# A dynamic convolution and a SwiGLU layer on one Trainium2 core: the first tile's work divided anew among the engines

## What is computed

```python
w = softmax(weight_gen, axis=-1)                     # 4 x 4096 x 8 heads x 7 taps
x_unf[b, s, k] = x_pad[b, s + k]                     # 6 rows of zeros ahead of each sequence
y = einsum('bshk,bskhg->bshg', w, x_unf)             # 4 x 4096 x 192, 24 columns to a head
xn = y / sqrt(mean(y * y, -1) + 1e-6) * rms_g        # 16384 x 192
g, val = xn @ w_gate, xn @ w_val                     # 192 x 1536 each
out = (g * sigmoid(g) * val) @ w_out                 # 1536 x 192
```

## Time and profile before

| | |
|---|---|
| median of 3 runs | 1282.7 us |
| the profiled execution | 1281.68 us |
| its span in the profile | 1279.7 us |
| PE, matmuls | 1261.2 us busy, 99% |
| PEld, weight loads | 1180.4 us, 92% |
| DVE | 1002.0 us, 78% |
| ACT | 662.6 us, 52% |
| POOL | 44.7 us, 3% |

### The profile page before, as it was taken

The page is one execution under the profiler, slowest core; times in us unless marked ns, Lnnn a source line. Parts: engine busy times, 40 slices in busy tenths (PEclk is TensorE's granted clock), DMA queues, the critical chain, the costliest instruction groups (busy, mean ns, idle before and its releaser), DMA issues.

```text
span 1279.7 us, 32479 instructions
## 1 busy us (share of the span) xinstructions
PE 1261.2 (99%) x13544; PEld 1180.4 (92%) x13544; DVE 1002.0 (78%) x1516; ACT 662.6 (52%) x1426; POOL 44.7 (3%) x75
## 2 busy tenths in 40 slices
PE   8999999999999999999999999999999999999998
PEld 7988999999999899999989999999999999999997
DVE  7998888878787887888877777877877877877643
ACT  4554555565446555445564455554455554455543
POOL 1000000000000000000000000000000000000000
PEclk9999999999999999999999999999999999999999
DMA  9011321211211212212212112111122122121010
GB/s 292 40 43 27 97 67 44 69 58 56 62 47 56 69 45 69 57 38 69 69 45 68 47 50 69 53 61 57 44 64 69 45 69 57 39 69 39 14 38 14
DMA packets 19734, 76.29 MB, mean 60 GB/s; under 512 B 3212, under 2 KB 4876, under 8 KB 19464
## 3 DMA queue, kind: packets, MB, share of 16 engines
q1 hardware_dynamic: 18764, 72.78, 18.8%
q10 hardware_dynamic: 828, 1.47, 0.5%
HBM read 38.06 MB, written 12.58 MB: 40 GB/s over the span
## 4 chain that ended last, share of the span: by engine, by line
PE 90%; DVE 4%; issue 2%; ACT 2%; DMA 1%; ACTq 0%; POOL 0%; DVEq 0%
PE up_ps L796 57%; PE out_ps L836 22%; PE out_ps L840 10%; DVE h L683 1%; DMA raw<-in_moe_w_val 1%; DVE prod L224 1%; DVE y L226 1%; DVE h_lo L703 1%; PE up_ps L745 1%; ACT silu L469 1%; ACT L469 0%; ACT L449 0%; PE up_ps L750 0%; DMA taps<-in_weight_gen 0%; DVE last L635 0%
## 5 line engine op out<-in xcount | busy, mean ns | idle before, releaser
L796 PE MATMUL up_ps<-xT,w_hi 64*128 64x512 f32 x4608 | 779.7, 390 | 4.3 <-DVE h L683 3.5
L796 PEld LDWEIGHTS up_ps<-xT,w_hi 64*128 64x128 f32 x4608 | 481.2, 184 | 51.4 <-issue 6.7
L796 PE MATMUL up_ps<-xT,w_lo 64*128 64x512 f32 x2304 | 476.1, 387 | 0.0
L836 PE MATMUL out_ps<-wo,h_hi 64*128 64x384 f32 x3072 | 456.0, 354 | 5.5 <-DVE last L635 1.6
L484 ACT ACTIVATE h_hi<-h 128x512 fp32r<-128x512 f32 x384 | 242.4, 631 | 338.8 <-DVE h L683 332.2
L683 DVE TENSOR_TENSOR h<-up_ps,silu 128x512 f32<-128x512 f32 x384 | 264.4, 688 | 194.0 <-ACT silu L469 191.7
L840 PE MATMUL out_ps<-wo,h_lo 64*128 64x192 f32 x3072 | 413.3, 247 | 0.0
L469 ACT ACTIVATE silu<-up_ps 128x512 f32<-128x512 f32 x384 | 228.5, 595 | 238.9 <-PE up_ps L796 232.2
L836 PEld LDWEIGHTS out_ps<-wo,h_hi 64*128 64x128 f32 x3072 | 322.6, 184 | 11.2 <-DVE last L635 2.4
L840 PEld LDWEIGHTS out_ps<-wo,h_lo 64*128 64x128 f32 x3072 | 327.3, 187 | 3.7
L703 DVE TENSOR_TENSOR h_lo<-h,h_hi 128x512 fp32r<-128x512 f32 x384 | 263.1, 685 | 34.9 <-ACT h_hi L484 34.6
(11 more groups left out here) (75 smaller groups left out, 301.5 us busy)
## 6 DMA issues: line engine op xcount, KB each, us to landing
x_buf<-in_x SPq DMA_DIRECT2D x30, 960.0 KB, 4.7
xT<-xT SPq DMA_DIRECT2D x90, 256.0 KB, 3.8
result<-last SPq DMA_DIRECT2D x32, 384.0 KB, 2.3
taps<-in_weight_gen SPq DMA_DIRECT2D x1, 3136.0 KB, 20.7
raw<-in_moe_w_gate SPq DMA_DIRECT2D x3, 384.0 KB, 8.6
raw<-in_moe_w_val ACTq DMA_DIRECT2D x3, 384.0 KB, 10.4
last<-in_moe_w_out SPq DMA_DIRECT2D x1, 1152.0 KB, 18.0
x_first<-in_x SPq DMA_DIRECT2D x2, 384.0 KB, 7.4
```

Source lines behind the costliest of these rows:

```text
L796: mm = nc.tensor.matmul(ps[:, banks, :], w[rows, s, cols], xT[rows, t, s, part, :], start=(at == 0), stop=ends)
L836: nc.tensor.matmul(out_ps[:, j, 0:2 * D], h_hi[rows, g % HB, cols], wo[rows, g, :, :].rearrange("p a d -> p (a d)"), start=(g == 0 and k < ...
```

## The change

- **DMA.** Gate, value and output weights are loaded in halves of columns (blocks), all of half 0 ahead of half 1. The gains come in three transfers instead of five, ahead of the value weights. Each half has its own semaphore.
- **Transposes that nobody reads.** 34 ahead of `sum_first` instead of 50, 34 behind it instead of 30, and 6 new ones (`WAIT_TURNS`) between `turn_x` of tile 0 and the first hidden block.
- **ACT at the start.** `w_high(0, 1)` goes ahead of the squares, `w_high(0, 2)` stays behind them.
- **PE.** The steps of hidden blocks 0 and 1 of tile 0 are interleaved, so that those which need low x come later.
- **POOL** takes the products with the last two taps of tile 1's convolution and their sum (`last_taps`), the low weights of half 1 for s = 0 and 1 (`w_low_pooled`) and those of the output weights' second half (`wo_low_pooled`). ACT scales the raw weights by the gains for it (`raw_times_gains`), since POOL's form is a plain subtraction.
- **DVE** is left with 10 instead of 13 steps in tile 0 and `w_low(1, 2)` alone in half 1; tile 1's squares and scales come one f earlier, and so does `scale_rest(1, 1)`. Four steps of tile 2's division of taps and two products move into f = 9 to 11 of tile 0. At tile 1 `out_low` and `out_add` come at f = 0 instead of 2.

```diff
-        WARM_TURNS, KEEP_TURNS = 50, 30
+        WARM_TURNS, KEEP_TURNS, WAIT_TURNS = 34, 34, 6
...
-        SECOND_DONE = NORM1_DONE + CONV
+        SECOND = CONV - 3
+        SECOND_DONE = NORM1_DONE + SECOND
...
-            def load_w(s):
-                c = CHUNKS[0][s]
-                sp.dma_start(raw[0:DB, s, :], w_gate[c * DB:(c + 1) * DB, :]).then_inc(w_loaded[s], 16)
+            def load_gate(n, s):
+                c, cols = CHUNKS[0][s], slice(n * F // 2, (n + 1) * F // 2)
+                sp.dma_start(raw[0:DB, s, cols], w_gate[c * DB:(c + 1) * DB, cols]).then_inc(w_loaded[n][s], 16)
+
+            def load_out(n):
+                fs = slice(n * FB // 2, (n + 1) * FB // 2)
+                sp.dma_start(raw_out[:, fs, :], w_out_d[:, fs, :]).then_inc(wo_loaded[n], 16)
...
             load_first(0)
-            load_w(0)
+            load_gate(0, 0)
             load_taps(1)
-            load_w(1)
-            load_w(2)
+            load_gate(0, 1)
+            load_gate(0, 2)
             load_first(1)
-            sp.dma_start(raw_out, w_out_d).then_inc(wo_loaded, 16)
+            load_out(0)
+            for s in range(SLOTS):
+                load_gate(1, s)
+            load_out(1)
...
+            def last_taps():
+
+                heads = lambda a: a.rearrange("p (q g) -> p q g", g=G)
+                pool.wait_ge(xfirst_loaded[1], 16)
+                pool.wait_ge(first_mix, NORM1_DONE)
+                for n, product in enumerate((prod_first, prod_pool)):
+                    k = K - 2 + n
+                    nc.gpsimd.tensor_tensor(heads(product[:]), heads(flat(x_first[:, J + k:J + k + J, :])),
+                                            tap_w[:, :, k].unsqueeze(2).to_broadcast([P, J * H, G]), ALU.mult).then_inc(pool_mix, 1)
+                pool.wait_ge(pool_mix, 2)
+                nc.gpsimd.tensor_tensor(prod_first[:], prod_first[:], prod_pool[:], ALU.add).then_inc(pool_mix, 1)
+
+            def w_low_pooled(s):
+                cols = slice(F // 2, F)
+                pool.wait_ge(raw_scaled, s + 1)
+                nc.gpsimd.tensor_tensor(w_lo[:, s, cols], raw[:, s, cols], w_hi[:, s, cols].bitcast(F32),
+                                        ALU.subtract).then_inc(w_lo_pooled, 1)
+
+            def wo_low_pooled():
+                fs = slice(FB // 2, FB)
+                pool.wait_ge(wo_hi_done, 2)
+                nc.gpsimd.tensor_tensor(wo[:, fs, 1, :], raw_out[:, fs, :], wo[:, fs, 0, :].bitcast(F32),
+                                        ALU.subtract).then_inc(wo_lo_done, 1)
+
             inverse_rms(0)
+            last_taps()
...
+            w_low_pooled(0)
...
+            w_low_pooled(1)
...
+            wo_low_pooled()
...
-            load_val(0)
-            act.dma_start(gains[:, 0:1], g_d[0:P, :]).then_inc(gains_loaded, 16)
...
+            with nc.allow_non_contiguous_dma(reason="192 gains, one to a partition"):
+                chunks = g_d.rearrange("(s c) a -> c (s a)", c=DB)
+                act.dma_start(gains[0:DB, :], chunks).then_inc(gains_loaded, 16)
+                act.dma_start(gains[DB:P, 0:SLOTS:2], chunks[:, 1:SLOTS]).then_inc(gains_loaded, 16)
+                act.dma_start(gains[DB:P, 1:2], chunks[:, 0:1]).then_inc(gains_loaded, 16)
+            for n in range(2):
+                for s in range(SLOTS):
+                    load_val(n, s)
...
+            def raw_times_gains(s):
+                cols = slice(F // 2, F)
+                nc.scalar.activation(raw[:, s, cols], raw[:, s, cols], ACT.Copy, scale=gains[:, s:s + 1]).then_inc(raw_scaled, 1)
...
+            w_high(0, 1)
             square(0, 0, range(J))
-            w_high(0, 1)
             w_high(0, 2)
...
-                squares_early, scales_early = {0: 10, 1: 7, 2: 6, 3: 3}.get(T), {0: 11, 1: 8}.get(T)
+                squares_early, scales_early = {0: 9, 1: 7, 2: 6, 3: 3}.get(T), {0: 10, 1: 8}.get(T)
...
-                    if f == 2 and not first:
+                    if f == (0 if T == 1 else 2) and not first:
                         out_low(T - 1)
...
                     if first and f in (1, 2, 3):
                         w_high(1, f - 1)
+                        if f < 3:
+                            raw_times_gains(f - 1)
...
             w_low(0, 0)
+            w_low(0, 1)
             scale_rest(0, 0)
-            w_low(0, 1)
             w_low(0, 2)
...
+                    if n == SECOND - 1:
+
+                        dve.wait_ge(pool_mix, 3)
+                        first_step(NORM1_DONE + n, nc.vector.tensor_tensor(flat(y[:, 1, :, :]), flat(y[:, 1, :, :]),
+                                                                           prod_first[:], ALU.add))
+                        continue
...
-            seconds = [1, 0, 1, 1, 1, 2, 2, 1, 2, 2, 0, 0]
+            seconds = [0, 1, 1, 1, 1, 2, 2, 2, 0, 0, 0, 0]
...
+            steps_early = {0: (None,) * 9 + ((2, 4), (2, 1), (2, 1)),
...
-                        if f in (2, 3, 4):
-                            w_low(1, f - 2)
-                        if f == 7:
-                            wo_low(1)
+                        if f == 4:
+                            w_low(1, 2)
...
-                    if first and f == xf:
+                    if first and f == xf - 1:
                         scale_rest(1, 1)
...
-                if T < 2 and f == 0:
+                if T == 0 and f < 2 or T == 1 and f == 0:
...
                 if first and f == FB // 2:
-                    pe.wait_ge(w_lo_done, 2 * SLOTS)
+                    pe.wait_ge(w_lo_done, SLOTS + 1)
+                    pe.wait_ge(w_lo_pooled, SLOTS - 1)
...
+                    if first and f == 0:
+
+                        hidden(T, t, 0, 0, 7)
+                        hidden(T, t, 1, 0, 4)
+                        hidden(T, t, 0, 7)
+                        hidden(T, t, 1, 4)
+                        continue
...
             turn_x(0, 0, 1)
+            for _ in range(WAIT_TURNS):
+                nc.tensor.transpose(up_ps[:, 0, 0, 0:P], ident[:], ident[:])
```

More of the change, by code:

```diff
@@ L109, in dynconv_swiglu @@
         gains_loaded = sem("gains_loaded")
-        w_loaded = [sem("w_loaded0"), sem("w_loaded1"), sem("w_loaded2")]
-        wo_loaded = sem("wo_loaded")
+        w_loaded = [[sem(f"w_loaded{n}{s}") for s in range(SLOTS)] for n in range(2)]
+        wo_loaded = [sem("wo_loaded0"), sem("wo_loaded1")]
         x_loaded = [sem("x_loaded0"), sem("x_loaded1")]
@@ L127, in dynconv_swiglu @@
         first_mix = sem("first_mix")
+        pool_mix = sem("pool_mix")
+        raw_scaled = sem("raw_scaled")
+        w_lo_pooled = sem("w_lo_pooled")
         y_summed = sem("y_summed")
@@ L361, in _, with load_val @@
             first_exps(0)
-            def load_val(s):
-                c = CHUNKS[1][s]
-                act.dma_start(raw[DB:P, s, :], w_val[c * DB:(c + 1) * DB, :]).then_inc(w_loaded[s], 16)
-            load_val(0)
-            act.dma_start(gains[:, 0:1], g_d[0:P, :]).then_inc(gains_loaded, 16)
-            for s in (1, 2):
-                for m in range(2):
-                    c = CHUNKS[m][s]
-                    act.dma_start(gains[m * DB:(m + 1) * DB, s:s + 1], g_d[c * DB:(c + 1) * DB, :]).then_inc(gains_loaded, 16)
-            load_val(1)
-            load_val(2)
+            def load_val(n, s):
+                c, cols = CHUNKS[1][s], slice(n * F // 2, (n + 1) * F // 2)
+                act.dma_start(raw[DB:P, s, cols], w_val[c * DB:(c + 1) * DB, cols]).then_inc(w_loaded[n][s], 16)
+            with nc.allow_non_contiguous_dma(reason="192 gains, one to a partition"):
[6 more added lines that the diff above has]
+                    load_val(n, s)
             def w_high(n, s):
-                if n == 0:
-                    if s == 0:
-                        act.wait_ge(gains_loaded, 80)
-                    act.wait_ge(w_loaded[s], 32)
+                if n == 0 and s == 0:
+                    act.wait_ge(gains_loaded, 48)
+                act.wait_ge(w_loaded[n][s], 32)
                 cols = slice(n * F // 2, (n + 1) * F // 2)
@@ L638, in _ @@
             second_norm()
-            seconds = [1, 0, 1, 1, 1, 2, 2, 1, 2, 2, 0, 0]
+            seconds = [0, 1, 1, 1, 1, 2, 2, 2, 0, 0, 0, 0]
             steps_other = [2, 1, 2, 2, 1, 1, 1, 1, 2, 1, 2, 1]
-            steps_early = {1: ((2, 2), (2, 2), (2, 1), (2, 2), (2, 2), (2, 2), (2, 2), None, (3, 4), None, (3, 1), (3, 2)),
+            steps_early = {0: (None,) * 9 + ((2, 4), (2, 1), (2, 1)),
[1 row of a table added]
                            2: ((3, 2), (3, 2), (3, 1), (3, 2), (3, 2), (3, 1, 4, 3), (4, 2), (4, 2), (4, 2), None, (4, 2), (4, 2)),
                            3: ((4, 2), (4, 2), (5, 3), (5, 3), (5, 1), (5, 2), (5, 1), None, (5, 2), (5, 1), (5, 2), (5, 2))}
-            steps_done = {2: NORM, 3: 0, 4: 0, 5: 0}
+            steps_done = {2: 0, 3: 0, 4: 0, 5: 0}
             early = {}
-            for T in (1, 2, 3):
+            for T in (0, 1, 2, 3):
```

(13 more changed lines are left out.)

9 lines of the change are left out of this document (7 added, 2 removed), and 1 row of the table steps_early.

## The result

The changed kernel took **1286.3 us** (median of 9 runs, 1285.37 to 1286.87) beside 1282.7 us for the kernel before in 9 runs of the same measurement: 1.0023 times as long, with a 95% interval of 1.0015 to 1.0032. Forecast were 1281.0 us and a gain of 1.7. So the sign is wrong, and the value lies above the range. The profiled execution took 1286.37 us, 4.7 more than the profiled one of before, which lay 1.0 under its median.

A forecast was written before the change was run, and what follows sets the result against it. PE was taken as the bound nearly throughout, with gains only where it falls behind its pace: 2.8 + 1.4 + 1.9 = 6.1 us, less 4.4 for POOL, gives 1.7 off 1282.7, so 1281.0; range 1275.6 to 1285.2.

The forecast's parts named there:

- tile 1's block 4 at 77.0: Start of tile 1's block 4 on PE: 77.0, which is 78.65 less the 1.7 us gain.
- The start: Start of tile 0: `turn_x` at 19.3 against 22.68, 3.4 us sooner; 2.8 us gained by block 4.
- The mechanism of the hold: DVE instructions with two SBUF inputs wait for POOL's instructions that read SBUF, as POOL waits for DVE's; assumed.
- Its price: P, a POOL instruction's time, taken as 1.4 us; 5P - 2.67 = 4.4 us lost ahead of `project(0)`.
- The rival of a high price: POOL's instructions hold DVE in f = 0 and 1 from P = 2.5 up; 1287.4 at 2.7; chance 0.12.
- The clock during the stall: PE's clock while it waits ahead of `project(0)` of tile 0: the prediction had no term for it.
- block 4 of tile 0 at 37.9: Start of tile 0's block 4 on PE, expected at 37.9 if the forecast is right; 36.29 before.
- four slow pairs at the start: First pairs of tile 0 at the low clock: about 1.7 us if not covered, costed at nothing.
- The last POOL instruction … is done well before: POOL's last instruction, and anything PE needs from POOL (block 6, `project(6)`), comes in time; no cost.
- PE stalls in f = 4 to 9, which I have at none: Blocks f = 4 to 9: PE never waits; stalls there would show the forecast wrong.
- The end of tile 0: Block 10's start to tile 1's start: 9.42 us instead of 10.83, 1.4 gained.
- Tile 1: Tile 1's blocks 0 to 3 and `project(0)`: 10.49 us instead of 12.43, 1.9 gained.

The follow-up runs named there:

- run 5: The changed kernel with the low half of the output weights for blocks 6 to 11 back on DVE at f = 7: 1284.75 us, 1.0014.
- run 2: The changed kernel with 40 more unread transposes ahead of `project(0)` of tile 0: 1285.31 us, 1.0022.
- the second kernel of run 9: The changed kernel without POOL's part, squares behind the first `w_hi`, one convolution step at tile 1's f = 0: 1279.83 us, 0.9975.
- runs 3 and 4: 3: changed kernel, POOL held until the second `h_lo`, 1284.46 us. 4: changed kernel without POOL's part, unused memsets and copies added on POOL, 1282.59 us.
- run 6: The changed kernel with 40 unread transposes ahead of `project(0)` and `wo_low(1)` back on DVE at f = 7: 1283.89 us, 1.0003.

## Why the prediction was wrong

The step that failed is the price of POOL's work: the forecast stopped at the wait of `project(0)`, took the work behind it at full speed, and put POOL's sixth instruction at nothing. I forecast tile 1's block 4 at 77.0; the trace has 83.08 (the medians differ by 5.3). The 6.1 us between, step by step:

- **The start**, "19.3 for `turn_x`": 20.03, **0.7 short**. The six pairs of sums ran nearly as forecast, from 7.7 to 15.5. I gave the second `w_hi` until 15.5 and looked only at its own load. But two `w_hi` of 0.94 stand back to back ahead of the squares, and the first could begin only at 14.32, so they end at 16.2. That first start varies from one profiled execution to the next, from 13.75 (run 5) to 16.39 (run 2). With only the first `w_hi` ahead of the squares (the second kernel of run 9) `turn_x` came at 19.20, as forecast.
- **The mechanism of the hold**, "I take it so": right. The changed kernel's rows and runs 3 and 4 show it; from the trace of before only POOL's side could be seen.
- **Its price**, P = 1.4 and 4.4 us: 1.55 for a product and 5.0 in all, **0.6 short**. It lies inside my bounds for P (0.95 to 2.1). By an estimate from the ratio of 1.96 of the Trainium skill, "GPSIMD Engine Reference", section 3.1, it would have been 1.87; the trace has 1.55 beside DVE's 0.95, 1.63 times. The rival of a high price, from P = 2.5, did not come true; the loss came out of other terms.
- **The clock during the stall**: no term at all, **2.5** (2.1 in `project(0)`, 0.4 in the pair behind it). I followed the hold to `project(0)` and stopped: "block 4 of tile 0 at 37.9" takes `project(0)` at full speed. I had even priced four slow pairs at the start. But in the forecast's own numbers PE was ready at 30.4 and began `project(0)` at 35.65, a stall of 5 us, longer than the one of 1.8 after which the earlier trace rows show 0.53. Run 2 gives 2.2 of them back.
- **"The last POOL instruction … is done well before"** and "PE stalls in f = 4 to 9, which I have at none": **1.45**. The sentence asked when PE needs POOL's result, not which DVE instruction POOL's would hold. It waited for ACT's high half, ran from 45.86, and held a product at f = 4 with PE close behind. Run 5 removes it.
- **The end of tile 0**, 9.42: 10.26, **0.8 short**. `turn_x` waited for nothing, as forecast, but the last `h_lo` came 0.99 us after it, not 0.34.
- **Tile 1**, 10.49: 10.44, right.

These are 0.7 + 0.6 + 2.5 + 1.45 + 0.8 = 6.05. Two thirds of it, 3.95, are consequences of a hold whose first link was right. With both taken out (run 6) the kernel is level with before, where I had it 1.7 faster. Its stretch from `turn_x` to tile 1's block 4 is 59.58 us where the forecast has 57.7; the 1.9 left are the price (0.6), the end of tile 0 (0.8) and the 0.33 that DVE's `wo_low(1)` costs at f = 7.
